# Moving the third weight pair's rounding to ScalarE and reordering GpSimd's splits in the first steps of a fused attention and two-layer MLP kernel

## What is computed

```python
kv  = einsum('bhsd,bhse->bhde', k, v)            # batch 4, 8 heads, 576 tokens, head size 64
out = einsum('bhsd,bhde->bhse', q, kv)
x   = out / sqrt(mean(out*out, -1) + 1e-6) * g_norm      # 2304 tokens x 512
h = x @ w_in                                     # 512 -> 2048
g = h * sigmoid(1.702 * h)
x = g @ w_out                                    # 2048 -> 512
h = x @ w_in2                                    # 512 -> 2048
g = max(h, 0) + log1p(exp(-abs(h)))
y = g @ w_out2                                   # 2048 -> 512
```

## Time and profile before

| | before |
|---|---|
| time, median of 3 runs | 817.43 us (816.87 to 817.56) |
| time of the profiled execution | 818.9 us |
| its span | 817.1 us |
| TensorE matmuls (PE) busy | 806.3 us, 99% |
| TensorE weight loads (PEld) busy | 735.5 us, 90% |
| VectorE (DVE) busy | 587.0 us, 72% |
| ScalarE (ACT) busy | 424.8 us, 52% |
| GpSimd (POOL) busy | 224.5 us, 27% |
| chain that ended last | PE 91%, DVE 4%, DMA 2% |

### The profile page before, as it was taken

How to read it: one execution, slowest core, us unless ns; L and a number is a source line. 1 busy time by engine, 2 the same in 40 slices (tenths; PEclk the granted TensorE clock), 3 DMA queues, 4 the chain that set the end, 5 groups by cost and what they waited for, 6 DMA issues and landing times.

```text
span 817.1 us, 12401 instructions
## 1 busy us (share of the span) xinstructions
PE 806.3 (99%) x4614; PEld 735.5 (90%) x4614; DVE 587.0 (72%) x1029; ACT 424.8 (52%) x809; POOL 224.5 (27%) x263
## 2 busy tenths in 40 slices
PE   8998999999999999999999999999999999999998
PEld 7887999999999999999998888898988988989886
DVE  3788767687665686665678777888767889766774
ACT  4772332334221233222246776688767678766765
POOL 4889887304422403263501401200000000000000
PEclk9999999999999999999999999999999999999999
DMA  9955536435455472756543535324433323452402
GB/s 357 406 191 186 229 143 267 172 116 206 163 224 180 164 249 91 241 200 254 228 161 114 206 100 205 109 90 148 167 124 117 154 91 99 159 181 90 147 35 78
DMA packets 24427, 139.80 MB, mean 171 GB/s; under 512 B 2224, under 2 KB 6960, under 8 KB 17200
## 3 DMA queue, kind: packets, MB, share of 16 engines
q1 hardware_dynamic: 24224, 138.95, 46.3%
q10 hardware_dynamic: 144, 0.07, 0.0%
HBM read 104.92 MB, written 34.08 MB: 170 GB/s over the span
## 4 chain that ended last, share of the span: by engine, by line
PE 91%; DVE 4%; DMA 2%; ACT 1%; issue 1%; SPq 0%; ACTq 0%; DVEq 0%
PE ps L660 42%; PE ps L728 24%; PE ps L736 15%; PE ps L733 8%; DMA kv_in_sb<-k_v 2%; DVE xs_f L1015 1%; DVE gs_f L1083 1%; DVE gs_f L1044 0%; DVE rms L984 0%; PE ps L601 0%; DVE gs L1097 0%; DVE gs L1093 0%; PE ps L584 0%; DVE ex L1106 0%; ACT rms L791 0%
## 5 line engine op out<-in xcount | busy, mean ns | idle before, releaser
L660 PE MATMUL ps<-xs,w_in 128*128 128x384 f32 x2016 | 410.3, 339 | 2.6 <-DVE gs_f L1044 2.3
L660 PEld LDWEIGHTS ps<-xs,w_in 128*128 128x128 f32 x2016 | 357.7, 188 | 27.5 <-DVE gs_f L1044 3.8
L728 PE MATMUL ps<-w_out,gs 128*128 128x512 f32 x864 | 226.1, 393 | 0.0
L1044 DVE TENSOR_TENSOR gs_f<-ps,gs_f 128x384 f32<-128x384 f32 x240 | 133.1, 555 | 115.9 <-PE ps L660 114.4
L728 PEld LDWEIGHTS ps<-w_out,gs 128*128 128x128 f32 x864 | 160.0, 188 | 24.1 <-issue 0.5
L736 PE MATMUL ps<-gs,w_out 128*128 128x512 f32 x576 | 148.7, 393 | 0.0
L736 PEld LDWEIGHTS ps<-gs,w_out 128*128 128x128 f32 x576 | 105.9, 188 | 16.4
L835 ACT ACTIVATE lg<-gs_f 128x384 f32<-128x384 f32 x73 | 38.3, 525 | 128.3 <-DVE gs_f L1044 127.6
L505 POOL TENSOR_TENSOR w_in<-w_in_f,w_in 128x256 fp32r<-128x256 f32 x112 | 95.3, 886 | 28.5 <-ACT w_in L877 28.2
L733 PE MATMUL ps<-gs,w_out 128*128 128x256 f32 x576 | 83.6, 281 | 0.9 <-issue 0.9
L872 ACT CAST gs<-gs_f 128x384 fp32r<-128x384 f32 x96 | 48.9, 509 | 67.7 <-DVE gs_f L1113 66.5
(11 more groups left out here) (64 smaller groups left out, 588.2 us busy)
## 6 DMA issues: line engine op xcount, KB each, us to landing
w_in<-w_kept SPq DMA_DIRECT2D x40, 1792.0 KB, 7.3
w_kept<-w_in SPq DMA_DIRECT2D x16, 1792.0 KB, 10.2
w_in_f<-w_in SPq DMA_DIRECT2D x16, 512.0 KB, 4.0
w_out_f<-w_out SPq DMA_DIRECT2D x16, 512.0 KB, 8.7
kv_in_sb<-k_v SPq DMA_DIRECT2D x8, 640.0 KB, 10.9
kv_in_sb<-k_v SPq DMA_DIRECT2D x8, 576.0 KB, 12.6
q_sb<-q_t SPq DMA_DIRECT2D x16, 288.0 KB, 11.0
out<-xy SPq DMA_DIRECT2D x18, 256.0 KB, 7.7
```

What stands on the lines that cost most here:

```text
L660: mm = nc.tensor.matmul(ps[:, bank, 0:HALF], w[:, wp, W_OF[k], cols], xs[:, k, xp, t], start=(new and t == 0 and (wp, xp) == (HI, HI)), st ...
L728: mm = nc.tensor.matmul(ps[:, acc_bank(1, j), 0:DM], g[:, j * P:(j + 1) * P], w, start=new, stop=done)
L1044: nc.vector.tensor_tensor(to, bank, other, ALU.add).then_inc(added, 1)
```

## The change

GpSimd no longer rounds pair 2 of w_in; ScalarE does (W_POOL = 2), as its first work of step 1, ahead of the sigmoid of C11. GpSimd waits for all four low parts of step 0 instead of two, and for that rounding, before it starts the low part of pair 2. In steps 1 to 5 GpSimd does the pair of w_out first, then the sums and the low part of w_in's pair m+2. On ScalarE pair 3 is rounded in step 2 after the sigmoid of C11 and the pair of w_out (before: in step 1, after the sigmoid of C22), and pairs 4 to 7 are rounded in steps 2 to 5 after the sigmoid of C22 (before: after that of C11 and the pair of w_out).

```diff
-    W_POOL = 3
+    W_POOL = 2
...
             w_out_low(0, 0)
             w_sums(2)
 
-
-            pool.wait_ge(g_split, C21 + 1)
-            w_high(2)
+            pool.wait_ge(g_split, TILES)
+            pool.wait_ge(w_hi_made, 1)
             w_low(2)
             for m in range(1, ALL):
...
+                if m < STEPS - 2:
+                    for pair, layer in w_out_of(m):
+                        w_out_low(pair, layer)
                 if d:
                     w_sums(d)
-                for pair, layer in w_out_of(m):
-                    w_out_low(pair, layer)
+                if m >= STEPS - 2:
+                    for pair, layer in w_out_of(m):
+                        w_out_low(pair, layer)
                 if d:
                     pool.wait_ge(w_hi_made, d - W_POOL + 1)
                     w_low(d)
...
-            LATE_ROUNDS = (1, STEPS)
+            LATE_ROUNDS = (2, 3, 4, 5, STEPS)
...
+                if m == 1:
+                    round_w_in(2)
                 if m > 0:
                     hidden(m, C11)
                 if m > 0:
                     for pair, layer in w_out_of(m):
                         round_w_out(pair, layer)
-                if split_at(m) and m not in LATE_ROUNDS:
+                if split_at(m) and m not in (0, 1) + LATE_ROUNDS:
                     round_w_in(split_at(m))
+                if m == 2:
+                    round_w_in(3)
```

## The result

| | before | the change |
|---|---|---|
| median of 9 executions | 817.43 us (816.87 to 818.33) | 820.18 us (818.94 to 821.16) |
| ratio | | 1.0029 (95% interval 1.0020 to 1.0038) |
| profiled execution, its span | 818.9, 817.1 us | 820.29, 818.4 us |

The change makes the kernel slower: the ratio is 1.0029, and the medians are 2.75 us apart. Between the two profiled executions the difference is only 1.4 us, and that the two numbers disagree is half of what there is to learn here.

The account below looks back on a forecast made before the run. TensorE's matmuls were taken as the bound (busy 99% of the span), so only its waits or low clock count. Terms -3.80 + 5.1 = +1.3 us on the 817.43 median gave 818.7 us, range 816.4 to 820.9.

Parts of the forecast that it names:

- Term 1: Step 1: TensorE's wait before P4 goes as VectorE's gates speed up; -3.80 us, 2.16 the wait and 1.64 the clock.
- Term 2: Step 3: a new relay through GpSimd and ScalarE makes P2 about 3.4 us late; +5.1 us with clock and U2.
- The wait at w_out: Step 3: the second multiplication waits 0.6 us for w_out's pair 2 from GpSimd.
- U2 as the second limit: Step 3: P7 waits for U2 behind VectorE's gate of C12, 4.5 us late at full clock.
- The rule on the shared ports: VectorE and GpSimd exclude each other; sums of pair 4 at 0.69 us each, 2.8 instead of 3.02, sum 0.2 us lower.
- The forecast's own range: Net +1.3 us for the whole kernel, with its own range of +0.2 to +2.3; chance 0.60.
- the slower rival: Step 3: a second or longer low-clock stretch costs 1.64 us more; net +2.9, 820.3 us; chance 0.25.
- The faster one: Step 3: the relay runs free at GpSimd's 4.84 us pace, without low clock; net -1.8, 815.6 us; chance 0.10.
- the gates would not speed up: Step 0: VectorE's long instructions have another cause than GpSimd; term 1 near zero, +5 us or more, 822.5; chance 0.05.

Follow-up runs that it names:

- the profile of 1: Profiled execution of the kernel before, run again unchanged: 817.71 us at mean clock 1.000; median 817.71 us, ratio 1.0003.
- e5: The change, run again unchanged, on a second chip: 819.86 us, ratio 1.0021 to the kernel before.
- e6: The change, with ScalarE rounding pair 3 right behind the copy of step 2's P1: 817.46 us, ratio 0.9993 to the kernel before.
- e7: The kernel before, with GpSimd waiting for all four low parts of step 0 and still rounding pair 2 itself: 821.79 us, ratio 1.0041.
- e2: The change, with ScalarE rounding pairs 4 to 7 behind the copy of P1 in the following step: 815.76 us, ratio 0.9970 to the kernel before.
- e3: The change, with GpSimd's sums of pair 4 made in its idle gap and ScalarE's roundings of pairs 3 and 4 moved: 814.92 us, ratio 0.9964.
- e4: As e2, but GpSimd waits for two low parts of step 0, not all four: 816.05 us, ratio 0.9975 to the kernel before.
- e8: e3 with GpSimd's sums of pair 2 after the gate of C21 and ScalarE's rounding of pair 2 behind C11's sigmoid: 815.99 us, ratio 0.9978.
- e9: e3 run again on a third chip: 815.17 us, ratio 0.9960 to the kernel before.
- e10: e3 with w_out's pair 0 rounded by ScalarE instead of GpSimd, before the root of unit 12: 815.15 us.
- e11: As e10, with ScalarE's rounding of w_out's pair 0 behind the root of unit 14: 814.71 us, ratio 0.9959 to the kernel before.
- e12: e3 run a third time, on a fourth chip: 815.50 us, ratio 0.9968 to the kernel before.

## Why the prediction was right, and what was wrong in it

**Term 1 as a mechanism: right.** VectorE's gates took 1.45 us each, U3 was in time, P4 had no wait, P1 of step 2 came at 75.22 for a forecast 75.07. Neither the low part of pair 2 nor w_out's pair 1 was late.

**Term 1 as a size: this is the step that failed.** I took -3.80 us, of which 1.64 were the low clock, and put the sum on the median of the runs. The low clock behind the wait is in 27 of 81 executions. In a median execution there is none to remove, and term 1 is 78.87 - 75.07 less 1.64, so 2.16; the profile of 1 has it at (77.45 - 62.49) - (75.22 - 62.54) = 2.28. There was a sign that I passed over: the profiled execution was 1.5 us above the median, as I wrote, and 1.5 us is about the price of the low clock. On the profiled executions themselves the sum came out: from the first second multiplication to P1 of step 2 the change gains (78.87 - 62.36) - (75.22 - 62.54) = 3.83 us, from there to P1 of step 4 it loses (111.67 - 75.22) - 2 x 15.74 = 4.97, together +1.1 us for a forecast +1.3.

**Term 2: right in its place, its chain and nearly its size.** Forecast: the copy ends at 98.05, P2 starts at 98.1; measured 98.12 and 98.17. The parts were off in both directions and cancelled: low part 5.20 between starts (6.09 taken), w_out 3.65 (3.12), sums 3.29 (3.02), together 12.14 against 12.23. The wait at w_out was 0.28 us, and the start there 0.43 us late, where 0.6 was forecast. U2 as the second limit at full clock (4.5 us) is confirmed by e5, whose P7 starts at 100.85, 4.4 us after its undisturbed place, and by e6. With the right clock term the steps give -2.2 + 4.5 = +2.3 us at full clock; measured 2.19 in the stretch (48.61 - 46.42) and 2.1 between the medians.

**The rule on the shared ports.** The sums of pair 4 were to run at the pace of 0.69 us once VectorE is idle. VectorE's last instruction before them, with both inputs in SBUF, is this one:

```profile
91.84 0.97 DVE L1105 TENSOR_TENSOR gs<-gs_f,gs 128x384 fp32r<-128x384 f32 x1
```

After its end, at 92.8, three of the sums took 0.74, 0.74 and 0.73 us at 0.70 us between starts; the first, still beside it, took 1.05. This agrees with the Trainium skill (SBUF — State Buffer, Who interferes with whom), by which an instruction of VectorE with two SBUF inputs contends with one of GpSimd that reads SBUF. But the sum had nothing to gain from it. The row from which I took 3.02 us already had the undisturbed pace (0.73 for the sum at 83.70), and the sums of pair 4 took 3.29 us to the start of the rounding, 0.27 more, because the first ran beside VectorE.

**Rivals and chances.** The forecast's own range was +0.2 to +2.3: the 2.75 us between the medians of the result lie above it, the 2.1 us at equal clock inside. The time lies inside the stated range (816.4 to 820.9), on the side to which I gave 0.40, not 0.50. That the range held it is in part luck: its upper part was there for the slower rival, whose 820.3 the median of 820.18 nearly meets for another reason. That rival named a second or a longer stretch at the low clock. Neither of the change's two profiles shows one; a longer one, 2.83 us dear, stands in e7, and two of the change's 20 executions have the mean clock of 0.996 that e7's slower ones have (821.12 and 821.16 us), but neither was profiled. The faster one needed a relay 1.5 us shorter; it was 0.1 us shorter. That the gates would not speed up fell with the first profile.

## What to carry to other kernels

When a rounding or a copy moves to an engine that is idle on average, look at what stands behind it in that engine's queue: here ScalarE was busy half of the time, and one instruction that waited for GpSimd held up the sigmoid and the copy on which TensorE depended, so that TensorE was 3.3 us late. The same work behind that copy, or fed by sums that were made in GpSimd's gap, left the kernel 1.7 to 2.9 us faster than before, where the change had made it 2.8 us slower. Price a change against one profiled execution only after asking whether that execution is a typical one: its distance to the median is a term of the sum. And a shared resource such as GpSimd beside VectorE is a reason to move work in time, not only between engines.

## What the runs showed that I had not expected

- The same wait of TensorE, 1.87 us in both profiles, is followed by the low clock in some executions and not in others. Without it, and with no other wait over 0.9 us in steps 1 to 5, the low clock did not come in any of the 64 executions of e2, e3, e4, e6, e8, e9, e10, e11 and e12 (mean clock 0.999 or 1.000 in all); behind a wait of 1.87 us it came in 27 of 81, of 2.6 us in 10 of 20, of 3.68 us in 5 of 5. What decides in a single execution is open.
- The price of the low clock is not fixed: 1.56 us between the two profiles of the kernel before, 2.83 us in e7, where it lasted longer.
- A low-clock stretch can be almost free: 0.52 us between the two profiles of the change, where VectorE's U2 would have been the next wait anyway.
- The attention part ends up to 1 us apart in executions of kernels that do not differ there (the 24 products before the wait start at 56.61 to 57.65 us in e12 and e4). Differences under 1 us between kernels had to be read from the stretch, not from the times.
